# Hashed attention with the scores computed twice: once for the row maximum, once transposed for the product with V

## Chip, cores, metric

One Trainium2 chip (trn2), one core of it. The metric is the time of one execution on the device in microseconds (us), lower is better. Engines are named as in the profile: PE (TensorE), PEld (its weight loads), DVE (VectorE), ACT (ScalarE), POOL (GpSimd), SP (SyncE, which here only issues DMAs; SPq is its queue).

## What is computed

```python
# attention: batch 2, 8 heads, seq 768, head_dim 64; proj is 64 x 6
q_bits = (q @ proj > 0);  k_bits = (k @ proj > 0)          # 6 hash bits each
mask = bucket(q_bits)[:, None] == bucket(k_bits)[None, :]
scores = where(mask, q @ k.T / 8, -1e9)
scores -= max(scores, axis=-1)
attn = exp(scores);  attn /= sum(attn, axis=-1) + 1e-9
x = attn @ v                                               # (1536 tokens, 512)
# then a dense layer with SoLU and layer norm (512 -> 1024 -> 512)
# then a mixture of 8 experts, one expert per token (512 -> 1024 -> 512)
```

The change touches the attention alone: 16 heads of 768 queries by 768 keys.

## The kernel before

**Precision.** The tensors are float32. A score is made of fp32r products: q and k are split in a high part (ACT, L1022 and L1023) and a low part, the remainder (POOL, L1230), and a score tile is the sum of A1·B1 (high·high and high·low, stacked on 128 partitions) and A2·B2 (low·high, and below it the hash rows). The hash rows are 12 rows a head, made of the signs of q·proj and k·proj (PE L444, then DVE L705) and scaled so that a pair of unequal buckets adds a huge negative number to its score. So the mask costs no instruction of its own. The four operands of a head are put together by ten SBUF to SBUF DMAs that SP issues (fill, L363 to L376), into two sets of buffers, c = 0 and 1, for even and odd heads.

**One head**, queries on partitions. For each of six query tiles j of 128 rows: PE computes the scores (L454, four matmuls of 384 columns into two PSUM banks, a "slot"; there are two slots), DVE takes the negated row maximum (L712) and from it the scale and the bias (L714, L716), and ACT writes the exponentials to SBUF and their row sum (L1017). After three tiles (a half w of the head) DVE takes the reciprocal of the three sums (L723, L725), and POOL multiplies the three 128x768 tiles by it (normalize, L1223). V's product needs the keys on partitions, so PE then transposes the half's 18 blocks of 128x128 (L464), in six groups of three, and ACT (L1029) and DVE (L735) copy these out of PSUM to PTb. Then PE computes V's product for the half (L477): V's 128x64 block is the stationary operand, and two runs of 192 queries go to partitions 0 to 63 and 64 to 127 of one bank. Each of these float32 matmuls stands in the trace as two records. DVE copies the result of a head into xT (attended, L740).

**Order.** Every engine's order is written out by hand in a function heads(i, left) that holds a pair of heads; pairs() runs it for the first pair, then in a hardware loop for pairs 1 to 5, then for the last two. Within it PE takes scores of head h+1 and h+2 between the transposes and products of head h. Beside the attention, each head also prepares one piece of the dense layer's weights: DMA to stg, multiplied by g_ln on DVE (L729), high part on ACT (L1033), low part on POOL (L1235).

**Around it.** The first two heads' scores and exponentials stand ahead of the loop. After the last head the dense layer runs (hidden, L498 to L500, on), then routing, then the experts (from about 530 us). Their first input is take(), which splits xT in high and low parts (ACT L1046, POOL L1240).

## Time and profile before

| | |
|---|---|
| time, median of 3 runs | 787.79 us (786.18 to 789.93) |
| the profiled execution: its own time, its span | 788.34 us, 786.5 us |
| PE busy, weight loads busy | 628.5 us (80%), 508.3 us (65%) |
| DVE, ACT, POOL busy | 423.3, 323.8, 272.4 us |
| mean granted clock of PE | 0.901 |

The span is the time from the first to the last instruction of the profiled execution. The granted clock is the share of TensorE's full speed (2.4 GHz) that it was given: 1.00 or 0.50 in any stretch, and something between in a mean.

### The profile page before, as it was taken

How to read it: one execution, taken by the hardware profiler on the slowest of the kernel's cores; microseconds unless marked ns; L12 is line 12 of the kernel's file. 1: busy time of each engine (PE TensorE's matmuls, PEld its weight loads, DVE VectorE, ACT ScalarE, POOL GpSimd, SP SyncE). 2: the span in 40 equal slices, each digit the busy share in tenths (PEclk: the TensorE clock that was granted, in tenths of full speed). 3: DMA queues.
4: the chain of work that ended last, by engine and by line, in shares of the span. 5: the costliest groups of instructions: out<-in, count | busy, mean ns of one | idle time of the engine just before them, and what ended most of it. 6: DMA issues, size and time to landing. Idle time of an engine off the chain costs nothing.

```text
span 786.5 us, 12094 instructions
## 1 busy us (share of the span) xinstructions
PE 628.5 (80%) x3574; PEld 508.3 (65%) x3575; DVE 423.3 (54%) x764; ACT 323.8 (41%) x531; POOL 272.4 (35%) x200
## 2 busy tenths in 40 slices
PE   0658686868777787777999999981089999999994
PEld 0446565656565666655888888861078878878883
DVE  2546666666757565714465656546333564646431
ACT  1445555555545455532222222233243455545520
POOL 2365556565656464532123232253400100000010
PEclk9779888898989898987999999995589999999998
DMA  4457834435252515001000000022661756566510
GB/s 132 119 134 210 240 106 96 119 71 143 63 151 56 156 43 135 24 1 70 38 1 0 0 0 0 1 62 112 230 239 43 247 176 206 186 214 211 176 30 26
DMA packets 39262, 83.86 MB, mean 107 GB/s; under 512 B 7485, under 2 KB 10429, under 8 KB 39232
## 3 DMA queue, kind: packets, MB, share of 16 engines
q1 hardware_dynamic: 31952, 72.30, 31.5%
q10 hardware_dynamic: 5040, 4.87, 2.4%
q0 software_dynamic: 2240, 6.31, 2.1%
q8 instruction: 17, 0.28, 0.1%
q14 instruction: 13, 0.11, 0.0%
HBM read 52.09 MB, written 12.35 MB: 82 GB/s over the span
## 4 chain that ended last, share of the span: by engine, by line
PE 61%; DVE 11%; issue 8%; ACT 6%; POOL 5%; SPq 4%; DMA 4%; ACTq 1%; DVEq 1%; POOLq 0%
PE PS L477 8%; PE PS L454 6%; PE PS L464 4%; PE PS L646 4%; PE PS L648 4%; PE PS L647 3%; PE PS L498 3%; PE PS L500 3%; PE PS L627 3%; PE PS L499 3%; PE PS L628 3%; PE PS L629 3%; PE PS L558 3%; PE PS L560 3%; PE PS L559 3%
## 5 line engine op out<-in xcount | busy, mean ns | idle before, releaser
L1223 POOL TENSOR_TENSOR at_P<-at_P,sb_rr 128x768 f32<-128x768 f32 x96 | 138.3, 1468 | 119.2 <-DVE sb_rr L725 119.2
L454 PE MATMUL PS<-at_B,at_A 128*128 128x384 f32 x384 | 105.1, 403 | 35.3 <-DMA at_B<-at_HB 19.0
L712 DVE TENSOR_REDUCE sb_nm<-PS 128x1 f32<-128x768 f32 x96 | 91.6, 954 | 75.2 <-PE PS L454 74.7
L464 PE MATMUL PS<-sb_cst,at_P 128*128 128x128 f32 x576 | 79.5, 286 | 54.3 <-ACT at_PT L1029 54.3
L1017 ACT ACTIVATE at_P<-PS,sb_nb,sb_sc 128x768 f32<-128x768 f32 x96 | 95.7, 1000 | 65.1 <-DVE sb_nb L716 65.1
L454 PEld LDWEIGHTS PS<-at_B,at_A 128*128 128x128 f32 x384 | 72.2, 216 | 57.8 <-ACT at_P L1017 23.6
L464 PEld LDWEIGHTS PS<-sb_cst,at_P 128*128 128x128 f32 x576 | 67.5, 144 | 62.4 <-ACT at_PT L1029 40.2
L941 DVE TENSOR_TENSOR at_W<-at_raw,at_W 128x2048 f32 (+1 forms) x30 | 68.0, 2290 | 70.6 <-ACT at_W L1093 67.9
L1314 POOL DMA_INDIRECT out<-at_yb,sb_to x16 | 15.8, 985 | 204.3 <-DVE at_yb L953 204.3
L1093 ACT ACTIVATE at_W<-at_raw 128x2048 f32 (+1 forms) x32 | 60.4, 1911 | 61.4 <-issue 32.8
L477 PE MATMUL PS<-at_PT,at_V 128*64 128x192 f32 x768 | 85.1, 381 | 0.7 <-DVE at_PT L735 0.7
L1029 ACT ACTIVATE at_PT<-PS 128x384 f32<-128x384 f32 x144 | 61.5, 488 | 39.9 <-PE PS L464 39.9
L477 PEld LDWEIGHTS PS<-at_PT,at_V 128*64 128x64 f32 x768 | 61.8, 163 | 23.9 <-issue 8.4
L1269 POOL TENSOR_TENSOR at_cn<-at_eb,sb_mv 128x1024 f32<-128x1024 f32 x12 | 22.7, 1894 | 108.0 <-DVE sb_mv L763 108.0
L646 PE MATMUL PS<-at_W,at_hTh 128*128 x128 | 51.5, 402 | 5.0 <-DVE at_hTl L972 4.8
L627 PE MATMUL PS<-at_W,at_xsh 128*128 x128 | 52.6, 411 | 3.2 <-DVE at_xsl L945 3.2
L628 PE MATMUL PS<-at_W,at_xsh 128*128 x128 | 51.0, 399 | 0.0
L629 PE MATMUL PS<-at_W,at_xsl 128*128 x128 | 50.9, 398 | 0.0
L648 PE MATMUL PS<-at_W,at_hTl 128*128 x128 | 50.0, 391 | 0.0
L647 PE MATMUL PS<-at_W,at_hTh 128*128 x128 | 49.9, 390 | 0.0
L498 PE MATMUL PS<-at_wsp,at_xch 128*128 128x512 f32 x96 | 41.2, 430 | 7.3 <-POOL at_xcl L1240 7.3
L735 DVE COPY at_PT<-PS 128x384 f32<-128x384 f32 x48 | 26.6, 554 | 34.2 <-PE PS L464 34.2
(145 smaller groups left out, 1062.8 us busy)
## 6 DMA issues: line engine op xcount, KB each, us to landing
at_raw<-w SPq DMA_DIRECT2D x32, 1024.0 KB, 5.5
at_A<-at_H SPq DMA_DIRECT2D x32, 192.0 KB
at_B<-at_H SPq DMA_DIRECT2D x32, 192.0 KB
rows_by_expert<-at_empty SPq DMA_DIRECT2D x19, 257.0 KB, 6.4
at_XS<-rows_by_expert ACTq DMA_DIRECT2D x17, 256.0 KB, 2.6
at_stg<-w_solu SPq DMA_DIRECT2D x16, 256.0 KB, 3.3
at_R<-qT SPq DMA_DIRECT2D x8, 384.0 KB, 3.3
at_R<-kT SPq DMA_DIRECT2D x8, 384.0 KB, 4.2
```

The costliest lines, as they stand in the source:

```text
L454: m = mm(slot(j)[:, g, :], a[c][:, j * P:(j + 1) * P], b[c][:, g * HALF:(g + 1) * HALF], start=(a is A1), stop=(a is A2))
L464: m = pe.transpose(PS[:, T0 + kt % 3, j * P:(j + 1) * P], Pr[c][w][j][:, kt * P:(kt + 1) * P], ident)
L477: m = mm(PS[g * D:(g + 1) * D, PVB, w * QQ:(w + 1) * QQ], V[c][:, kt, :], PTb[w][:, kt, g * QQ:(g + 1) * QQ], start=(kt == 0), stop=(kt == ...
L627: mm(PS[:, g, :], xsh[:, x_k], W[:, high], start=(k == 0), stop=False)
L628: mm(PS[:, g, :], xsh[:, x_k], W[:, low], start=False, stop=False)
L629: m = mm(PS[:, g, :], xsl[:, x_k], W[:, high], start=False, stop=(k == KB - 1))
L646: mm(PS[:, 4 + c, :], hTh[:, h_f], W[:, high], start=(f == 0), stop=False)
L647: mm(PS[:, 4 + c, :], hTh[:, h_f], W[:, low], start=False, stop=False)
L648: m = mm(PS[:, 4 + c, :], hTl[:, h_f], W[:, high], start=False, stop=(f == FB - 1))
L712: dve.tensor_reduce(nm[:, col], slot(j), AX.XY, ALU.max, negate=True).then_inc(s_nm, 1)
L1017: fn(Pr[c][w][j % UT].rearrange("p (g n) -> p g n", g=2), slot(j), ACT.Exp, bias=nb[:, col], scale=sc[:, col], accum_out=sm[:, col]).then_ ...
L1223: pool.tensor_tensor(p, p, rr[:, col].broadcast_to([P, S]), ALU.mult).then_inc(s_norm, 1)
```

## The change

The scores of a head are computed in two forms.

1. leading(h, j), queries on partitions, six tiles: one product of the high parts with the hash rows stacked below (76 partitions, two matmuls of 384 columns a tile instead of four). DVE takes the negated row maximum as before (maximum), and that is all that is done with these scores.
2. maxima zeroes the maxima of rows without a partner, turn_maxima transposes the six columns of a head on PE, and place_maxima (DVE) writes them, less their sign, into six rows of A1 against rows of ones in B1.
3. products(h, kt), keys on partitions, six tiles of 128 keys: A1 and B1 (102 partitions: high parts, hash rows, maxima) and A2 and B2 (128 partitions: the two mixed products), for each half g of the queries into its own PSUM bank. So the maximum is already subtracted, and ACT's exponential (128x384, a constant scale, no bias, no sum) writes PT in the form that V's product reads. The transposes, their copies out of PSUM and POOL's multiplications are gone.
4. The row sums: POOL adds up the six PT tiles (add, five instructions a head), and sums multiplies the total by ones on PE, which leaves the sum in all 64 partitions. DVE takes 1/(sum + 1e-9) of 128x384 values (inverse) and scales V's product by it (attended). One more column in PT and V's product (385 instead of 384) carries a small term, mu, that is added to it.

V's product runs in two parts of three key tiles, (0, 1, 2) behind a head's own products and (3, 4, 5) in the middle of the next head. There are four sets of operands instead of two, filled three heads ahead (fill, still ten DMAs a head; at the start ACT issues half of them); R and HB are double. The scaling of the dense layer's weights by g_ln moves from DVE to ACT. The hardware loop over pairs becomes sixteen heads written out. The rows of zeros that SP writes to HBM in one run after the first pair now go two a head.

The core of the diff:

```diff
-QQ = UQ // 2
+SETS = 4
+ROWS1 = D + BITS
+MAXROW = 96
+ROWS = MAXROW + TILES
...
+        (PT,), w = many("PT", w, 1, KT * 2 * (HALF + 1))
+        PT = PT.rearrange("p (k g q) -> p k g q", k=KT, g=2)
+        w = (w + 7) // 8 * 8
+        acc, w = many("acc", w, 2, S)
+        (rec,), w = many("rec", w, 1, HALF)
...
+        STB, PVB, RB = 4, 6, 7
...
+            def fill(h):
+                sp.wait_ge(s_high, 2 * (h // 2) + 2)
+                sp.wait_ge(s_bits, h // 2 + 1)
+                wait(sp, s_st, 2 * KT * (h - SETS + 1))
+                for n in range(2):
+                    fill_1(sp, h, n)
+                sp.wait_ge(s_low, h // 2 + 1)
+                for n in range(2):
+                    fill_2(sp, h, n)
+            def load_v(h):
+                wait(sp, s_rb, h - 1)
+                sp.dma_start(V[h % 2], vP[h:h + 1].rearrange("o p (k d) -> p (o k) d", k=KT)).then_inc(ld_v[h % 2], 16)
...
+            def leading(h, j):
+                t, _, _ = set_of(h)
                 if j == 0:
-                    wait(pe, ld_f[c], FILL * p + FILL)
-                wait(pe, s_exp, 6 * h + j - 1)
-                for a, b in ((A1, B1), (A2, B2)):
+                    ready_1(pe, h)
+                wait(pe, s_nm, TILES * h + j - 1)
+                for g in range(2):
+                    m = mm(slot(h, j)[:, g, :], A1[t][0:ROWS1, j * P:(j + 1) * P],
+                           B1[t][0:ROWS1, g * HALF:(g + 1) * HALF], start=True, stop=True)
+                m.then_inc(s_slot, 1)
+            def turn_maxima(h):
+                pe.wait_ge(s_mm, h + 1)
+                m = pe.transpose(PS[0:TILES, RB, 0:P], mm_[:, h % 2 * TILES:(h % 2 + 1) * TILES], ident)
+                m.then_inc(s_mt, 1)
+            def products(h, kt):
+                t, _, _ = set_of(h)
+                if kt == 0:
+                    ready_2(pe, h)
+                    pe.wait_ge(s_mc, h + 1)
+                at_k = slice(kt * P, (kt + 1) * P)
+                for g in range(2):
+                    at_g = slice(g * HALF, (g + 1) * HALF)
+                    wait(pe, s_exp, 2 * (KT * h + kt) + g - 1)
+                    mm(PS[:, STB + g, 0:HALF], B1[t][0:ROWS, at_k], A1[t][0:ROWS, at_g], start=True, stop=False)
+                    mm(PS[:, STB + g, 0:HALF], B2[t][:, at_k], A2[t][:, at_g],
+                       start=False, stop=True).then_inc(s_st, 1)
+            def values(h, kts):
+                pe.wait_ge(s_exp, 2 * (KT * h + kts[-1]) + 2)
+                if kts[0] == 0:
+                    pe.wait_ge(ld_v[h % 2], 16 * (h // 2) + 16)
+                    wait(pe, s_fin, h)
+                for kt in kts:
                     for g in range(2):
-                        m = mm(slot(j)[:, g, :], a[c][:, j * P:(j + 1) * P], b[c][:, g * HALF:(g + 1) * HALF],
-                               start=(a is A1), stop=(a is A2))
-                m.then_inc(s_slot, 1)
-            def transposes(h, c, w, kts):
-                for kt in kts:
-                    if kt == 0:
-                        wait(pe, s_norm, 3 * (2 * h + w) + 3)
-                    wait(pe, *(evac_count(kt - 3, h, w) if kt >= 3 else evac_count(kt + 3, h - 1 + w, 1 - w)))
-                    for j in range(UT):
-                        m = pe.transpose(PS[:, T0 + kt % 3, j * P:(j + 1) * P],
-                                         Pr[c][w][j][:, kt * P:(kt + 1) * P], ident)
-                    m.then_inc(s_tr, 1)
-            def values(h, c, p, w):
-                wait(pe, *evac_count(ON_ACT[w][-1], h, w))
-                wait(pe, *evac_count(ON_DVE[w][-1], h, w))
-                if w == 0:
-                    wait(pe, ld_v[c], 16 * p + 16)
-                    wait(pe, s_pvev, h)
-                for kt in range(KT):
-                    for g in range(2):
-                        m = mm(PS[g * D:(g + 1) * D, PVB, w * QQ:(w + 1) * QQ], V[c][:, kt, :],
-                               PTb[w][:, kt, g * QQ:(g + 1) * QQ],
+                        m = mm(PS[g * D:(g + 1) * D, PVB, 0:HALF + 1], V[h % 2][:, kt, :], PT[:, kt, g, :],
                                start=(kt == 0), stop=(kt == KT - 1))
                 m.then_inc(s_pv, 1)
+            def sums(h):
+                pe.wait_ge(s_acc, (KT - 1) * (h + 1))
+                wait(pe, s_rec, 3 * h - 1)
+                for g in range(2):
+                    m = mm(PS[g * D:(g + 1) * D, RB, 0:HALF], cst[:, C_ONE:C_ONE + D],
+                           acc[h % 2][:, g * HALF:(g + 1) * HALF], start=True, stop=True)
+                m.then_inc(s_rb, 1)
...
+            for h in range(HEADS):
+                for kt in range(KT):
+                    ahead = (h + 1, kt + TILES - 2) if kt < 2 else (h + 2, kt - 2)
+                    if ahead[0] < HEADS:
+                        leading(*ahead)
+                    products(h, kt)
+                    if kt == 2:
+                        if h + 1 < HEADS:
+                            wait(pe, s_rec, 3 * h - 4)
+                            pe.wait_ge(s_bits, min(PAIRS, 2 + (h + 1) // 2))
+                            turn_maxima(h + 1)
+                        if h > 0:
+                            values(h - 1, (3, 4, 5))
+                            if h + 1 < HEADS:
+                                pe.wait_ge(s_mc, h + 2)
+                            sums(h - 1)
+                values(h, (0, 1, 2))
+                if h % 2 == 0 and h // 2 + 2 < PAIRS:
+                    wait(pe, s_rec, 3 * h - 1)
+                    hashes(h // 2 + 2, RB)
+            hidden(0, 0, 0, True)
+            values(HEADS - 1, (3, 4, 5))
+            sums(HEADS - 1)
+            hidden(0, 0, 1, True)
...
+            def maximum(h, j):
+                col = h % 2 * TILES + j
+                dve.wait_ge(s_slot, TILES * h + j + 1)
+                dve.tensor_reduce(nm[:, col:col + 1], slot(h, j), AX.XY, ALU.max, negate=True).then_inc(s_nm, 1)
+            def maxima(h):
+                cols = slice(h % 2 * TILES, (h % 2 + 1) * TILES)
+                dve.wait_ge(s_nm, TILES * h + TILES)
+                wait(dve, s_mt, h - 1)
+                dve.scalar_tensor_tensor(out=mm_[:, cols], in0=nm[:, cols], scalar=BIG / 2, in1=nm[:, cols],
+                                         op0=ALU.is_lt, op1=ALU.mult).then_inc(s_mm, 1)
+            def place_maxima(h):
+                dve.wait_ge(s_mt, h + 1)
+                dve.tensor_tensor(A1[h % SETS][MAXROW:ROWS, :].rearrange("p (j q) -> p j q", j=TILES),
+                                  PS[0:TILES, RB, 0:P].unsqueeze(1).broadcast_to([TILES, TILES, P]),
+                                  ident[0:TILES, 0:TILES].unsqueeze(2).broadcast_to([TILES, TILES, P]),
+                                  ALU.mult).then_inc(s_mc, 1)
+            def inverse(h):
+                dve.wait_ge(s_rb, h + 1)
+                dve.tensor_copy(mu[:, h % 2:h % 2 + 1], PS[:, PVB, HALF:HALF + 1]).then_inc(s_rec, 1)
+                dve.tensor_scalar(rec, PS[:, RB, 0:HALF], EPS, None, ALU.add).then_inc(s_rec, 1)
+                dve.wait_ge(s_rec, 3 * h + 2)
+                dve.reciprocal(rec, rec).then_inc(s_rec, 1)
+            def attended(h):
+                p, c = h // 2, h % 2
+                dve.wait_ge(s_rec, 3 * h + 3)
                 for g in range(2):
-                    m = dve.tensor_copy(
-                        xT[c * D:(c + 1) * D, ds(i * S, S)].rearrange("p (w g q) -> p w g q", w=2, g=2)[:, :, g, :],
-                        PS[g * D:(g + 1) * D, PVB, 0:UQ].rearrange("p (w q) -> p w q", w=2))
-                m.then_inc(s_pvev, 1)
+                    mine = slice(g * D, (g + 1) * D)
+                    m = dve.scalar_tensor_tensor(
+                        out=xT[c * D:(c + 1) * D, p * S + g * HALF:p * S + (g + 1) * HALF], in0=PS[mine, PVB, 0:HALF],
+                        scalar=mu[mine, c:c + 1], in1=rec[mine, :], op0=ALU.add, op1=ALU.mult)
+                m.then_inc(s_fin, 1)
...
+            for h in range(HEADS):
+                if h + 1 < HEADS:
+                    maximum(h + 1, TILES - 2)
+                    maximum(h + 1, TILES - 1)
+                    maxima(h + 1)
+                if h % 2 == 1 and h // 2 + 2 < PAIRS:
+                    hash_bits(h // 2 + 2, RB)
+                if h + 2 < HEADS:
+                    maximum(h + 2, 0)
+                if h + 1 < HEADS:
+                    place_maxima(h + 1)
+                if h > 0:
+                    inverse(h - 1)
+                if h + 2 < HEADS:
+                    maximum(h + 2, 1)
+                if h > 0:
+                    attended(h - 1)
+                if h + 2 < HEADS:
+                    maximum(h + 2, 2)
+                    maximum(h + 2, 3)
+            inverse(HEADS - 1)
+            attended(HEADS - 1)
...
+            def weights_of(h, kt, g):
+                act.wait_ge(s_st, 2 * (KT * h + kt) + g + 1)
+                if h > 0 and g == 0:
+                    act.wait_ge(s_pv, 2 * h - 1 if kt < 3 else 2 * h)
+                    act.wait_ge(s_acc, (KT - 1) * (h - 1) + max(kt, 1))
+                fn(PT[:, kt, g, 0:HALF], PS[:, STB + g, 0:HALF], ACT.Exp, scale=SCALE).then_inc(s_exp, 1)
...
+            for h in range(HEADS):
+                weights_of(h, 0, 0)
+                weights_of(h, 0, 1)
+                if h % 2 == 1 and h // 2 + 2 < PAIRS:
+                    high_parts(h // 2 + 2)
+                weights_of(h, 1, 0)
+                weights_of(h, 1, 1)
+                weights_scaled(h)
+                weights_of(h, 2, 0)
+                weights_of(h, 2, 1)
+                if h == HEADS - 1:
+                    act.wait_ge(s_rows0, 16 * SLOTS)
+                weights_high(h)
+                for kt in (3, 4, 5):
+                    weights_of(h, kt, 0)
+                    weights_of(h, kt, 1)
...
+            def add(h, kt):
+                total = acc[h % 2].rearrange("p (g q) -> p g q", g=2)
+                pool.wait_ge(s_exp, 2 * (KT * h + kt) + 2)
+                if kt == 1:
+                    wait(pool, s_rb, h - 1)
+                else:
+                    pool.wait_ge(s_acc, (KT - 1) * h + kt - 1)
+                pool.tensor_tensor(total, PT[:, 0, :, 0:HALF] if kt == 1 else total, PT[:, kt, :, 0:HALF],
+                                   ALU.add).then_inc(s_acc, 1)
...
+            for h in range(HEADS):
+                if h % 2 == 1 and h // 2 + 2 < PAIRS:
+                    low_parts(h // 2 + 2)
+                add(h, 1)
+                weights_low(h)
+                for kt in range(2, KT):
+                    add(h, kt)
```

## Rows read from the trace of the kernel before

**Rows 1.** Page: busy us (share of the span) and instructions of each engine.
```profile
PE 628.5 (80%) x3574; PEld 508.3 (65%) x3575; DVE 423.3 (54%) x764; ACT 323.8 (41%) x531; POOL 272.4 (35%) x200
```

**Rows 2.** Windows: stretch, length, engines' busy us (instructions), clock, DMA share, GB/s.
```profile
76.70:117.70 41.00, 31.98 (x228) 25.45 (x224) 24.96 (x57) 22.02 (x46) 23.27 (x17) 0.88 0.66 179
117.70:158.50 40.80, 31.62 (x228) 24.77 (x228) 25.98 (x57) 22.01 (x46) 23.42 (x17) 0.87 0.41 103
...
381.00:520.00 139.00, 137.64 (x710) 116.02 (x710) 86.11 (x140) 38.17 (x54) 38.41 (x32) 1.00 0.00 0
```

**Rows 3.** Waits in three turns, 76.7 to 199.4: total, times, longest.
```profile
POOL at_P L1223 <- DVE sb_rr L725: 42.5, 13, 5.4
...
PE PS L464 <- ACT at_PT L1029: 22.7, 6, 5.5
```

**Rows 4.** Groups by form, same turns: count, busy us, mean ns, idle before.
```profile
L1223 POOL TENSOR_TENSOR at_P<-at_P,sb_rr 128x768 f32<-128x768 f32 x37 | 53.3, 1466 | 42.5 <-DVE sb_rr L725 42.5
L454 PE MATMUL PS<-at_B,at_A 128*128 128x384 f32 x144 | 38.7, 395 | 4.8 <-ACT at_P L1017 4.7
L1017 ACT ACTIVATE at_P<-PS,sb_nb,sb_sc 128x768 f32<-128x768 f32 x36 | 35.9, 1000 | 16.3 <-DVE sb_nb L716 16.3
L712 DVE TENSOR_REDUCE sb_nm<-PS 128x1 f32<-128x768 f32 x36 | 34.4, 954 | 20.6 <-PE PS L454 20.5
L477 PE MATMUL PS<-at_PT,at_V 128*64 128x192 f32 x288 | 32.2, 384 | 0.0
L464 PE MATMUL PS<-sb_cst,at_P 128*128 128x128 f32 x216 | 30.2, 288 | 22.7 <-ACT at_PT L1029 22.7
...
L1029 ACT ACTIVATE at_PT<-PS 128x384 f32<-128x384 f32 x54 | 23.0, 488 | 12.9 <-PE PS L464 12.9
L1230 POOL TENSOR_TENSOR at_R<-at_R,at_H 128x768 fp32r<-128x768 f32 x6 | 10.8, 1827 | 5.1 <-ACT at_H L1022 5.1
...
L740 DVE COPY at_xT<-PS 64x384 f32 x12 | 6.7, 556 | 1.9 <-PE PS L477 1.6
...
L1022 ACT ACTIVATE at_H<-at_R 128x768 fp32r<-128x768 f32 x3 | 2.5, 832 | 0.0
```

**Rows 5.** Timeline of TensorE in one turn: start us, us, engine, line.
```profile
140.64 0.65 PEld L454 LDWEIGHTS PS<-at_B,at_A 128*128 128x128 f32 x4 [0.28 <-issue]
140.64 0.97 PE L454 MATMUL PS<-at_B,at_A 128*128 128x384 f32 x4
...
145.10 1.82 PEld L477 LDWEIGHTS PS<-at_PT,at_V 128*64 128x64 f32 x24 [0.25 <-ACT at_PT L1029]
```

**Rows 6.** Groups by form, whole span: the three sizes of reciprocal.
```profile
L725 DVE RECIPROCAL sb_rr<-sb_se 128x3 f32<-128x3 f32 x32 | 5.6, 176 | 1.1
...
L757 DVE RECIPROCAL sb_rs<-sb_se 128x1 f32<-128x1 f32 x12 | 2.0, 164 | 0.4
...
L868 DVE RECIPROCAL sb_r<-sb_r 128x12 f32<-128x12 f32 x1 | 0.2, 228 | 0.3 <-ACT sb_r L1123 0.3
```

**Rows 7.** Timeline 368 to 373 us: a short VectorE instruction beside a GpSimd one.
```profile
370.45 1.90 POOL L1269 TENSOR_TENSOR at_cn<-at_eb,sb_mv 128x1024 f32<-128x1024 f32 x1
370.59 1.77 DVE L768 TENSOR_TENSOR sb_var_all<-sb_var_all,sb_rs 128x1 f32<-128x1 f32 x1
```

**Rows 8.** Windows around TensorE's long wait in a turn.
```profile
150.00:152.50 2.50, 0.00 (x0) 0.00 (x0) 2.47 (x4) 0.80 (x2) 1.29 (x1) 1.00 0.96 358
...
153.70:157.10 3.40, 3.40 (x17) 2.31 (x17) 1.79 (x4) 2.10 (x6) 0.12 (x1) 0.50 0.00 0
```

**Rows 9.** Timelines: first ten fills' first and last; first scores; second hidden tile.
```profile
12.07 1.20 SPq L371 DMA_DIRECT2D at_A<-at_H  x2
...
19.09 0.71 SPq L376 DMA_DIRECT2D at_B<-at_HB  x1
...
21.12 2.93 PE L454 MATMUL PS<-at_B,at_A 128*128 128x384 f32 x8 [12.76 <-DMA at_B<-at_HB]
...
370.75 0.77 PE L498 MATMUL PS<-at_wsp,at_xch 128*128 128x512 f32 x1 [4.73 <-POOL at_xcl L1240]
```

427 lines of the change are left out of this document (140 added, 287 removed).

## Prediction, made before the changed kernel was run

> **What bounds the kernel now.** I read the page first, then windows by stage, the waits, the groups by form and the timeline of one turn. The page shows no engine full: PE 80%, DVE 54%, ACT 41%, POOL 35% of the span [rows 1]. The stages tell why that mean misleads. From 381 to 520 us, in the dense layer, PE is busy 137.6 of 139 us at clock 1.00: nothing there is touched. In the attention, one turn of the loop (two heads) takes 40.8 us, in which PE is busy 31.6, DVE 26.0, POOL 23.4, ACT 22.0, at a mean clock of 0.87 [rows 2]. So a head takes 20.4 us and nothing is saturated: it is a chain that goes round the engines. The waits give its links [rows 3]: POOL waits 42.5 us in three turns for the reciprocal, and PE waits 22.7 us, in pieces up to 5.5 us, for ACT's copies of the transposes. These idle stretches cost a second time: behind 2.5 us without a matmul, PE ran 3.4 us at clock 0.50 [rows 8]. What the change is worth is therefore the new length of a head, against 20.4.
>
> **What goes.** Per head, from three turns [rows 4]: 36 transposes (30.2/6 = 5.0 us of PE), nine copies on ACT and three on DVE, six multiplications on POOL (53.3/6 = 8.9 us), and the step maximum, bias, exponential, reciprocal, multiply, transpose, copy. The new order has no such round between a head's scores and its weights, except for the maxima, which are a head ahead.
>
> **What PE has now, full clock.** Four score matmuls take 0.65 us of loads and 0.97 us to their last end, so 0.163 each and a tail of 0.32 [rows 5]. leading: 12 x 0.163 = 1.95; products: 24 x 0.163 = 3.9. V's product streams 12 x 385 columns where 24 x 192 were streamed; half of it took 1.82 [rows 5], so three key tiles take 1.9, with the gap of 0.28 ahead of the next matmul 2.2, twice 4.4. sums is a sixth of V's product, 0.64. Turning the maxima 0.15; the hash products of a pair stream 384 columns four passes deep side by side, so as sums 0.64 with tail and gap, half a pair: about 0.5. V's product and sums are float32, and their two column halves run side by side as now. Sum 11.5, against about 14 before.
>
> **The pace of products.** Each bank is written by two matmuls, read by an exponential, and written again. Two matmuls 0.33, tail 0.32, exponential, 0.06 to PE's next. The exponential of 128x384 is not in the trace: a copy of that form takes 488 ns, an exponential of twice that 1000 [rows 4]. I take 0.53. So 1.24 us a key tile, while PE has 0.98 of work in it. ACT has six pairs of exponentials and three to four other instructions, some 7.5 us a head: not a bound, but the high parts of q and k (2 x 0.83 [rows 4]) stand between two exponentials in every odd head: 0.6 on average.
>
> **DVE.** Six maxima x 0.954 [rows 4], maxima 0.2, place_maxima about 0.95 (768 columns, as L712), hash bits 0.35, mu 0.15, the addition of 1e-9 from PSUM 0.6 (as L740), attended 2 x 0.57 [rows 4], and the reciprocal of 128x384. This one is the unknown. Its three sizes took 164, 176 and 228 ns for 1, 3 and 12 columns [rows 6]: 5.8 ns a column over both steps, so 0.164 + 383 x 0.0058 = 2.4 us. The lower bound is the rate of the other DVE rows, 1.04 ns a column: 0.56 us. Upper bound 3.3, if the slope at few columns flatters it. I take 2.4. DVE then has 11.7 us a head.
 The slope here is nearer to 5.6 cycles; by the page's figure the stall below is 0.8 us longer and the forecast some 11 us later.
>
> **POOL.** Five additions a head of two full 128x768 tiles. The nearest row is the low part, 1827 ns [rows 4], not the multiplication by a broadcast column, 1466; 9.1 us (7.3 by the other). With the low parts 1.8 and the weights' low part about 1.25: 12.2 us. The additions end some 8 to 11 us behind the point T below, sums needs them at about 14: hidden, if a head takes over 13 us.
>
> **SP.** Still ten fills a head: the first ten went out from 12.07 to 19.80 us, 0.77 each [rows 9]. 7.7 us a head, plus three loads and for ten heads two rows of zeros: under 11, and asked for more than a head ahead. No cost.
>
> **A full head, walked.** T = 0 is the end of sums(h-1). What is queued on DVE behind it decides: maximum(h+2, 1) stands behind inverse, and leading(h+2, 3) on PE waits for that maximum. DVE: tail 0.32, mu, addition, reciprocal with starts between 3.3, maximum 0.97: 4.6. PE meanwhile has only key tiles 3 and 4, until 2.2: it stalls 2.4 us. Key tile 5 until 5.6; V's product waits for attended (4.6 + 1.15 = 5.75) and ends at 8.0; hash products 0.5; key tiles 0 and 1, 2.5, high parts 0.6; key tile 2 and the turned maxima 1.1; V's product 2.2; sums 0.64. Sum 15.6. place_maxima is ready about 14.0, sums at 14.9: hidden, with 0.9 us to spare.
> The clock: 2.4 us of stall is near the 2.5 us that half clock followed [rows 8], but the other gaps of a head are 0.3 us or less. I take a half-clock stretch of 3.4 us in half of the heads; it does half of its work, so 1.7 us are lost each time: 0.8 a head. A full head: 16.4 us.
>
> **The sum.** First scores: operands for the maximum need no low parts (2 x 1.83 earlier) and three DMAs issued by SP beside three by ACT, not ten: about 13 us instead of 21.1 [rows 9]. Six maxima, turning and placing: products of head 0 at 22, some 3 us for head 2's operands: 25. Head 0 has no sums and no stall (six key tiles 7.4, V's product 2.2, turning 0.15, hash products 1.1): 10.9. Heads 1 to 13: 13 x 16.4 = 213. Heads 14 and 15 have no leading tiles and so no stall for them (7.4, V's product twice 4.4, sums 0.64, turning 0.15, and 1.1 in which V's product waits for attended): 2 x 13.7 = 27.4. That is 276.5. Then the tail: one half of the hidden tile (12 matmuls of 512 columns at the rate of the score matmuls) 2.6, V's product 2.2, sums 0.64, inverse and attended 4.8, take(), two thirds of L1022 on ACT and of L1230 on POOL, 2.0: the second hidden tile starts at 289 instead of 370.7 [rows 9]. 82 us less. The rest is unchanged: 788.3 - 82 = 706 for the profiled execution's own time (span 786.5 and 1.8 around it); the median was 0.5 under that execution, so 706 again.
>
> **Rivals.**
> **A, the division is cheap** (0.56 us): the stall goes from 2.4 to 0.55, and with it the half clock; 13 x (1.85 + 0.6) and 2 in the rest, so 34 less: 672. For it: only sizes of up to 12 columns are seen. Against it: both steps of the slope agree.
> **B, DVE and POOL block each other.** For it: L768, of 128x1, took 1.77 us and ended with a POOL instruction of 1.90 that had started before it [rows 7]. POOL will be busy three quarters of a head. maxima reads two operands in SBUF as L768 does, and the reciprocal reads and writes SBUF. Waiting for the addition in progress is up to 1.8 us, 0.9 on average, at each; on the path in the reciprocal, half so in maxima: 1.4 a head, with POOL's own delay up to 2.5. 13 x 1.4 to 13 x 2.5: 724 to 739. Against: POOL has 2 to 4 us of room.
> The Trainium skill ("SBUF — State Buffer", SBUF: two separate sides) says so: VectorE with two SBUF inputs, or in a 2-port mode, and GpSimd lock each other out for a whole instruction. The row agrees.
> **C, slower than before: PE never regains its clock.** Its work between exponentials is 0.98 of every 1.24 us, then a stall. If this pace is too low for the granted clock all along, the head's 11.5 us of PE become about 22, with what is left of the stall 23.4: 7 x 13, 8 and 15 at the ends, 114 more: 820. It decides from some 72% of the attention at half clock (82/114). Against it: after the half-clock stretch, which PE filled, the clock came back [rows 8], and at half clock PE is always full.
> The Trainium skill ("TensorE: Matmul & The Clock Gate", A second HAM failure mode: psum-queue depth-cycling) tells of a kernel that cycles through PSUM banks, idles briefly between groups and oscillates between the clocks; the oscillation is in my 0.8, the steady low clock is C.
>
> **How the numbers follow.** Forecast 0.50 (690 to 722), A 0.20 (655 to 690), B 0.22 (722 to 745), C 0.04, and 0.04 for something else that eats the gain, a product of V whose two halves no longer overlap (12 x 385 columns one after another: 4 us a head) or operands that come late. The range takes A and B: 666 to 742. Under 0.5% a measurement here can hardly tell from no change, about 4 us. Faster 0.94, same 0.01, slower 0.05.
>
> **What would show it.** One RECIPROCAL of 128x384 a head, at 2.4 us; PE waiting about 2.4 us for DVE's L712 once a head; no PE wait on ACT over 0.7 us but in odd heads; POOL's additions at 1.8 us and never waited for by sums; maxima stretched where POOL works; a head of 15.5 to 16.5 us; clock in the attention 0.85 to 0.95; second hidden tile at about 289 us. It is wrong if the stall in PE is elsewhere (sums behind POOL, products behind place_maxima), or if the head's length is set by ACT.

## The result and the profile after

| | before | changed |
|---|---|---|
| time, median of 4 runs on one chip | 787.21 us (786.18 to 789.93) | 710.52 us (709.01 to 714.1) |
| ratio, 95% interval | | 0.9027 (0.8985 to 0.907) |
| the profiled execution: own time, span, mean clock | 788.34, 786.5 us, 0.901 | 709.71, 707.6 us, 0.925 |

The change made the kernel 9.7% faster. The forecast was 706 us, in a range of 666 to 742.

The page of the changed kernel: busy time of the engines, the chain that ended last, two groups.

```profile
PE 598.6 (85%) x2886; PEld 440.4 (62%) x2887; DVE 400.0 (57%) x525; ACT 259.0 (37%) x403; POOL 268.5 (38%) x188
...
PE 70%; DVE 13%; issue 4%; DMA 3%; ACT 3%; POOL 2%; SPq 2%; ACTq 1%; DVEq 0%; POOLq 0%
...
L1242 POOL TENSOR_TENSOR at_acc<-at_acc,at_PT 128x768 f32<-128x768 f32 x64 | 107.6, 1681 | 14.8 <-ACT at_PT L1027 10.3
...
L754 DVE RECIPROCAL at_rec<-at_rec 128x384 f32<-128x384 f32 x16 | 40.9, 2553 | 0.5
```

Against [rows 1], PE lost 30 us of work, DVE 23, ACT 65, POOL 4, and none of them was full. The gain of 79 us in the span is thus mostly idle time. Line numbers have moved: leading is L472, turn_maxima L478, products L491 and L492, values L503, sums L512, the maximum L730, maxima L737, place_maxima L743, inverse L751 (mu), L752 (1e-9) and L754 (reciprocal), attended L762, the exponential L1027, high_parts L1036, low_parts L1231, add L1242, take L1252, hidden L533 to L535.

I cut the attention at each start of L751, which stands right behind sums, so that a stretch is one head. Windows of the changed kernel, with the columns of [rows 2]: three heads, one idle stretch of PE in the third, and what follows it.

```profile
116.02:130.10 14.08, 12.44 (x66) 7.78 (x67) 10.94 (x14) 6.26 (x14) 11.30 (x9) 1.00 0.94 235
130.10:146.09 15.99, 13.42 (x74) 8.05 (x75) 11.56 (x14) 7.61 (x16) 11.28 (x7) 1.00 0.46 123
146.09:161.73 15.64, 14.00 (x66) 8.60 (x67) 10.93 (x13) 6.37 (x14) 11.28 (x9) 0.89 0.95 231
148.56:150.17 1.61, 0.00 (x1) 0.00 (x1) 1.61 (x3) 0.50 (x2) 1.47 (x2) 1.00 1.00 217
150.50:153.90 3.40, 3.40 (x12) 2.00 (x12) 2.57 (x4) 0.98 (x2) 3.11 (x3) 0.50 1.03 307
```

A head takes 14.08 us, or 15.99 with the hash products and high parts of a pair, at full clock. With one stretch of half clock (3.4 us at 0.50, as in [rows 8]) it is 1.6 longer: the third row is a short head. From the first start of L751, 52.64, to the thirteenth, 242.61, there are 12 heads of 15.83 us on average, against 20.4 [rows 2]: seven of the short kind and five of the long one, with seven half-clock stretches among them.

The waits from 100 to 250 us, some ten heads:

```profile
DVE sb_nm L730 <- PE PS L472: 20.6, 9, 3.5
PEld PS L472 <- DVE sb_nm L730: 20.2, 11, 2.0
DVE sb_mu L751 <- PE PS L512: 17.8, 10, 1.8
PE PS L472 <- DVE sb_nm L730: 16.4, 10, 1.6
...
PE PS L491 <- ACT at_PT L1027: 3.5, 4, 0.9
```

POOL's wait for a reciprocal and PE's for ACT's copies [rows 3] are gone. PE now has one long wait a head, ten times 1.6 us, for a maximum. The timeline shows where it comes from. Below are first PE's rows, then DVE's, of the changed kernel around 116 us; sums of one head ends at 115.97, the point T of the prediction.

```profile
115.16 0.81 PE L512 MATMUL PS<-at_acc,sb_cst 128*64 128x384 f32 x4
115.91 0.62 PE L472 MATMUL PS<-at_B,at_A 76*128 76x384 f32 x2
...
120.10 0.62 PE L472 MATMUL PS<-at_B,at_A 76*128 76x384 f32 x2 [1.64 <-DVE sb_nm L730]
...
121.36 2.16 PE L503 MATMUL PS<-at_PT,at_V 128*64 128x385 f32 x12
...
129.24 0.81 PE L512 MATMUL PS<-at_acc,sb_cst 128*64 128x384 f32 x4
```

```profile
116.02 0.16 DVE L751 COPY sb_mu<-PS 128x1 f32<-128x1 f32 x1 [1.80 <-PE PS L512]
116.10 0.55 DVE L752 TENSOR_SCALAR at_rec<-PS 128x384 f32<-128x384 f32 x1
116.68 2.55 DVE L754 RECIPROCAL at_rec<-at_rec 128x384 f32<-128x384 f32 x1
119.15 0.89 DVE L730 TENSOR_REDUCE sb_nm<-PS 128x1 f32<-128x768 f32 x1
119.97 1.23 DVE L762 SCALAR_TENSOR_TENSOR at_xT<-PS,sb_mu,at_rec 64x384 f32<-64x384 f32 x2
```

DVE sits idle for 1.80 us until sums is done. Then mu, the addition and the division hold it for 3.1 us. The scores of tile 1, which ended at 116.53, wait behind them for their maximum, and PE, which needs their banks for tile 3, runs out of work at 118.46.

Groups by form of the changed kernel, 100 to 250 us: mean ns behind the busy time.

```profile
L1242 POOL TENSOR_TENSOR at_acc<-at_acc,at_PT 128x768 f32<-128x768 f32 x40 | 67.2, 1681 | 9.7 <-ACT at_PT L1027 7.2
L730 DVE TENSOR_REDUCE sb_nm<-PS 128x1 f32<-128x768 f32 x57 | 53.0, 944 | 22.2 <-PE PS L472 20.6
L1027 ACT ACTIVATE at_PT<-PS 128x384 f32<-128x384 f32 x114 | 50.1, 491 | 85.6 <-PE PS L492 85.3
```

The additions on POOL are somewhat shorter than the low parts of [rows 4], the maximum is as it was, and the exponential of 128x384 takes as long as a copy of that form did.

### The profile page after: what moved, and what is told of

It is laid out like the page before. It is cut to its first block, busy times and chain, and to the rows that moved or that the text cites. A ratio compares the mean times of both kernels' runs of the same rounds, so it can differ in the third digit from the quotient of the medians.

```text
span 707.6 us, 9729 instructions
## 1 busy us (share of the span) xinstructions
PE 598.6 (85%) x2886; PEld 440.4 (62%) x2887; DVE 400.0 (57%) x525; ACT 259.0 (37%) x403; POOL 268.5 (38%) x188
## 4 chain that ended last, share of the span: by engine, by line
PE 70%; DVE 13%; issue 4%; DMA 3%; ACT 3%; POOL 2%; SPq 2%; ACTq 1%; DVEq 0%; POOLq 0%
PE PS L503 11%; DVE at_rec L754 6%; PE PS L664 5%; PE PS L666 4%; PE PS L665 4%; PE PS L645 4%; PE PS L646 3%; PE PS L647 3%; PE PS L491 3%; PE PS L533 3%; PE PS L535 3%; PE PS L578 3%; PE PS L534 3%; PE PS L472 3%; PE PS L580 3%
## 5 line engine op out<-in xcount | busy, mean ns | idle before, releaser
L1027 ACT ACTIVATE at_PT<-PS 128x384 f32<-128x384 f32 x192 | 84.6, 491 | 135.2 <-PE PS L492 134.3
L730 DVE TENSOR_REDUCE sb_nm<-PS 128x1 f32<-128x768 f32 x96 | 89.2, 947 | 43.7 <-PE PS L472 41.3
L1242 POOL TENSOR_TENSOR at_acc<-at_acc,at_PT 128x768 f32<-128x768 f32 x64 | 107.6, 1681 | 14.8 <-ACT at_PT L1027 10.3
L503 PE MATMUL PS<-at_PT,at_V 128*64 128x385 f32 x384 | 80.0, 557 | 3.1 <-DVE at_xT L762 2.7
L472 PE MATMUL PS<-at_B,at_A 76*128 76x384 f32 x192 | 58.6, 394 | 28.0 <-DVE sb_nm L730 23.3
L491 PE MATMUL PS<-at_A,at_B 102*128 102x384 f32 x192 | 73.9, 385 | 9.5 <-ACT at_PT L1027 9.5
L472 PEld LDWEIGHTS PS<-at_B,at_A 76*128 76x128 f32 x192 | 34.4, 205 | 54.9 <-DVE sb_nm L730 31.8
L492 PE MATMUL PS<-at_A,at_B 128*128 128x384 f32 x192 | 67.3, 350 | 0.0
L503 PEld LDWEIGHTS PS<-at_PT,at_V 128*64 128x64 f32 x384 | 29.1, 152 | 40.4 <-issue 34.4
L491 PEld LDWEIGHTS PS<-at_A,at_B 102*128 102x128 f32 x192 | 37.5, 195 | 26.6 <-ACT at_PT L1027 20.4
L533 PE MATMUL PS<-at_wsp,at_xch 128*128 128x512 f32 x96 | 39.9, 416 | 6.2 <-POOL at_xcl L1252 6.2
L754 DVE RECIPROCAL at_rec<-at_rec 128x384 f32<-128x384 f32 x16 | 40.9, 2553 | 0.5
```

The lines of the kernel that those rows point to most:

```text
L472: m = mm(slot(h, j)[:, g, :], A1[t][0:ROWS1, j * P:(j + 1) * P], B1[t][0:ROWS1, g * HALF:(g + 1) * HALF], start=True, stop=True)
L491: mm(PS[:, STB + g, 0:HALF], B1[t][0:ROWS, at_k], A1[t][0:ROWS, at_g], start=True, stop=False)
L503: m = mm(PS[g * D:(g + 1) * D, PVB, 0:HALF + 1], V[h % 2][:, kt, :], PT[:, kt, g, :], start=(kt == 0), stop=(kt == KT - 1))
L730: dve.tensor_reduce(nm[:, col:col + 1], slot(h, j), AX.XY, ALU.max, negate=True).then_inc(s_nm, 1)
L754: dve.reciprocal(rec, rec).then_inc(s_rec, 1)
L1027: fn(PT[:, kt, g, 0:HALF], PS[:, STB + g, 0:HALF], ACT.Exp, scale=SCALE).then_inc(s_exp, 1)
```

## The experiments

The theory tested by e1, e2, e3 and e10 is that of the prediction: the chain on DVE behind sums costs a stall of PE in each head, and this stall some of the clock. e5, e6 and e9 test the place of the high and low parts, e7 the load of GpSimd, e4 and e8 another engine for the division. "PE busy" and "clock" below are from windows from 62 to 238 us, 176 us inside the attention; the last column is the number of stretches of half clock in it, 3.4 us each where nothing else is said.

| kernel | median us | ratio to before (95%) | PE busy, clock | half-clock stretches |
|---|---|---|---|---|
| changed | 710.52 | 0.9027 (0.8985 to 0.907) | 153.3, 0.94 | 6 |
| e1, short division | 671.68 | 0.8546 (0.8513 to 0.8579) | 170.2, 1.00 | 0 |
| e2, division split | 703.10 | 0.8949 (0.8918 to 0.898) | 152.4, 0.98 | 2 |
| e5, high parts late | 698.70 | 0.8885 (0.8852 to 0.8917) | 156.0, 0.94 | 6 |
| e7, short additions | 711.00 | 0.9053 (0.9015 to 0.909) | 153.4, 0.94 | 6 |
| e3, sums first | 673.90 | 0.8559 (0.8521 to 0.8596) | 169.6, 1.00 | 0 |
| e4, exp(-ln) on ACT | 700.03 | 0.8903 (0.8851 to 0.8954) | 156.2, 0.97 | 3 |
| e6, e3 and e5 | 693.13 | 0.8794 (0.8755 to 0.8834) | 162.0, 0.92 | 4 of 6.8 us |
| e8, e4 and e5 | 700.27 | 0.8912 (0.8848 to 0.8976) | 155.0, 0.95 | 5 |
| e9, e3, head 1 as in e5 | 676.06 | 0.8598 (0.8572 to 0.8624) | 169.9, 0.99 | the end of one |
| e10, maximum first | 727.34 | 0.925 (0.9221 to 0.928) | 147.8, 0.91 | 9 |

The kernel before took 785.88 us beside the first four (e1, e2, e5, e7), 787.09 beside the next four, 786.90 beside the last two.

### e1_short_division: what the division costs

```diff
-                dve.reciprocal(rec, rec).then_inc(s_rec, 1)
+                dve.reciprocal(rec[:, 0:12], rec[:, 0:12]).then_inc(s_rec, 1)
```

Only 12 of 384 columns are divided; all waits and all other work stay.

> The changed kernel with the reciprocal cut from 384 to 12 columns (the other 372 are left as sums, so the output is not scaled there): 2.55 us become about 0.23. Theory 1 (VectorE's chain behind sums, up to attended, sets the length of a head): PE's waits of 1.64 us for L730 go, V's product follows key tile 5 at once, a head falls from 15.7 to about 13.4 us, and the time from 710 to about 678 (675 to 683). Theory 2 (the division is beside the path, PE's own work and the exponentials set the length): within 3 us of 710. Theory 3 (POOL takes over as soon as the division is short): a head of about 14.5, time 692 to 700, with PE's L512 waiting for POOL.

Measured: 39 us under the changed kernel, 3 more than the range of theory 1 allowed (675 to 683); theories 2 and 3 are out. Two heads of e1, cut at L751:

```profile
105.22:117.56 12.34, 12.34 (x66) 7.72 (x67) 8.66 (x14) 6.26 (x14) 11.31 (x9) 1.00 0.93 228
117.56:131.66 14.10, 13.24 (x74) 7.84 (x75) 9.24 (x14) 7.61 (x16) 11.27 (x7) 1.00 0.71 175
```

They take 12.34 and 14.10 us instead of 14.08 and 15.99: 1.8 a head at full clock, and there is no half-clock stretch left, which is 0.95 more (seven short and five long heads at full clock are 14.88 on average in the changed kernel, and 15.83 was measured). Twelve heads take 156.9 us instead of 190.0, 33 less; 6 more come between the thirteenth start of L751 and the second hidden tile. In the short head PE has no idle time at all.

### e2_division_split: the same work in another order

```diff
-                dve.reciprocal(rec, rec).then_inc(s_rec, 1)
+                dve.reciprocal(rec[:, 0:HALF // 2], rec[:, 0:HALF // 2])
+            def inverse_rest(h):
+                dve.reciprocal(rec[:, HALF // 2:HALF], rec[:, HALF // 2:HALF]).then_inc(s_rec, 1)
...
                     maximum(h + 2, 1)
                 if h > 0:
+                    inverse_rest(h - 1)
                     attended(h - 1)
```

> The changed kernel with the reciprocal in two halves of 192 columns and maximum(h+2, 1) between them; the same work in another order. Theory 1a (two waits end together: leading's for this maximum and V's product's for attended): the wait of PE for L730 falls from 1.64 to about 0.4 us, a wait for DVE's L762 of about the same size appears ahead of V's product, and the time stays at 710, within 3 us. Theory 1b (the queue position of this one maximum is the whole cost): 1.3 us a head less, time 692 to 696.

Measured: 7 us under the changed kernel. The waits of e2, 100 to 250 us:

```profile
PE PS L503 <- DVE at_xT L765: 13.1, 10, 1.3
PEld PS L472 <- DVE sb_nm L730: 10.6, 15, 0.8
```

The stall is moved, as expected: less for the maximum, and 1.3 us a head for attended, which V's product needs. At full clock a head is no shorter (14.25 and 16.05 us against 14.08 and 15.99). I had expected no change within 3 us, and missed: two short waits in the place of one of 1.6 us left two half-clock stretches instead of six. Four times 1.6 is 6.4 of the 7 us. All four executions of e2 had a mean clock of 0.946 to 0.948, those of the changed kernel 0.922 to 0.935. By that count it was the shape of the stall, and not its sum, that made the difference, through the clock; why two short waits have fewer such stretches behind them is not shown.

### e10_maximum_first: the whole division behind the maximum

```diff
-                if h > 0:
-                    inverse(h - 1)
                 if h + 2 < HEADS:
                     maximum(h + 2, 1)
                 if h > 0:
+                    inverse(h - 1)
                     attended(h - 1)
```

> The changed kernel with maximum(h+2, 1) moved ahead of inverse(h-1) in VectorE's queue, nothing else. Theory 1a (leading's wait and V's product's wait for attended end together): PE's wait for L730 of 1.64 us goes, but the division starts about 0.6 to 0.9 us later, so V's product waits some 2.5 us for L762 and a head is 0.3 to 0.9 us longer: 712 to 722. Theory 1b (that maximum's place is the cost): 1.6 us a head less, 685 to 691.

Measured: 17 us slower than the changed kernel, 5 more than theory 1a allowed (712 to 722), and theory 1b is out. The waits of e10, 100 to 250 us:

```profile
DVE sb_nm L730 <- PE PS L472: 43.4, 17, 3.5
PEld PS L503 <- issue: 43.3, 89, 2.7
...
PE PS L503 <- DVE at_xT L762: 21.5, 9, 2.4
```

PE's wait for the maximum is gone and a longer one, 2.4 us, stands before V's product, with a stretch of half clock in nearly every head. A short head at full clock takes 14.80 us instead of 14.08, as theory 1a had it; what it had not counted are the added half-clock stretches (9 instead of 6 in the 176 us). The remedy that suggests itself, to serve the waiting engine first, made it worse: the division only delays another thing that PE needs.

### e3_sums_first: both waits taken away

PE computes sums(h-1) behind key tile 1 and not between V's product and key tile 3; DVE does the division behind the last maxima of the next head, and V's product of head h-1 follows it while DVE divides.

```diff
+                    if kt == 1:
+                        pe.wait_ge(s_bits, min(PAIRS, 2 + (h + 1) // 2))
+                        if h > 0:
+                            sums(h - 1)
                     if kt == 2:
...
                             values(h - 1, (3, 4, 5))
-                            if h + 1 < HEADS:
-                                pe.wait_ge(s_mc, h + 2)
-                            sums(h - 1)
...
+                if h % 2 == 1 and h // 2 + 2 < PAIRS:
+                    hash_bits(h // 2 + 2, RB)
                 if h + 1 < HEADS:
                     maximum(h + 1, TILES - 2)
                     maximum(h + 1, TILES - 1)
                     maxima(h + 1)
-                if h % 2 == 1 and h // 2 + 2 < PAIRS:
-                    hash_bits(h // 2 + 2, RB)
-                if h + 2 < HEADS:
-                    maximum(h + 2, 0)
-                if h + 1 < HEADS:
-                    place_maxima(h + 1)
                 if h > 0:
                     inverse(h - 1)
                 if h + 2 < HEADS:
+                    maximum(h + 2, 0)
                     maximum(h + 2, 1)
                 if h > 0:
                     attended(h - 1)
+                if h + 1 < HEADS:
+                    place_maxima(h + 1)
```

mu is copied in attended instead of inverse, V's load waits for V's product instead of sums, and some counts that PE waits for are adapted. No work is left out.

> The same work as the changed kernel in another order: on PE sums(h-1) directly behind products(h, 1), ahead of the turned maxima and the second part of V's product; on DVE the reciprocal directly behind maxima(h+1), so that it runs beside V's product, then maximum(h+2, 0) and (h+2, 1), attended (with mu), place_maxima. Theory (it is the place of the division in DVE's queue, not DVE's total of 11.7 us): PE's stall goes although the division is whole; heads of 12.6 and 14.4 us, as with the short division, with up to 0.8 us of waiting for GpSimd's last addition in every second head; time 674 to 685. Rival (DVE is too full for any order): stall at another place of DVE's queue, time 700 or more.

Measured: 673.90 us, 14.4% under the kernel before and 37 us under the changed one, at the lower edge of what was expected. It is the fastest full version here. Its windows, cut at sums:

```profile
100.35:114.22 13.87, 12.77 (x67) 7.61 (x66) 12.09 (x15) 8.50 (x19) 13.17 (x9) 1.00 0.70 169
114.22:127.53 13.31, 13.31 (x73) 7.86 (x74) 11.20 (x13) 5.57 (x13) 9.40 (x6) 1.00 0.85 221
```

PE is busy for the whole of the second and for 92% of the first, at full clock throughout, though each division still takes 2553 ns. DVE does more per microsecond than before (11.2 to 12.1 us of work a head). What cost the time was the division's place in the order, in DVE's queue and behind sums on PE, and not DVE's load; which of the two moves does how much was not tried apart. PE now bounds the second kind of head. In the first kind it waits 1.10 us once, ahead of sums: the profile names no releaser, but the addition on GpSimd that sums needs ends at 114.12 (rows below, under rival B) and sums starts at 114.22. So GpSimd, which was hidden before, now costs about a microsecond in every second head (five such waits between 20 and 250 us). The row of this wait in the timeline of PE:

```profile
114.22 0.87 PE L512 MATMUL PS<-at_acc,sb_cst 128*64 128x384 f32 x4 [1.10 <-issue]
```

### e7_short_adds: is GpSimd hidden?

```diff
+                n = HALF if kt < 3 else 8
-                pool.tensor_tensor(total, PT[:, 0, :, 0:HALF] if kt == 1 else total, PT[:, kt, :, 0:HALF],
-                                   ALU.add).then_inc(s_acc, 1)
+                pool.tensor_tensor(total[:, :, 0:n], PT[:, 0, :, 0:n] if kt == 1 else total[:, :, 0:n],
+                                   PT[:, kt, :, 0:n], ALU.add).then_inc(s_acc, 1)
```

The row sums lack most of key tiles 3 to 5.

> The changed kernel with GpSimd's additions of key tiles 3 to 5 cut to 8 of 384 columns of each half (so the row sums lack half of the tiles): GpSimd has some 4.5 us less work a head. Theory (GpSimd is hidden, 2 us or more of room, and it doesn't slow VectorE): within 3 us of 710, PE never waits for GpSimd in either. Rival (the additions delay the exponentials or VectorE's work through the ports): 8 us or more are gained.

Measured: POOL's work from 62 to 238 us falls from 122.3 to 74.4 us, and the time stays, as expected (711.00 against 710.52), with the same PE busy time, clock and number of half-clock stretches. GpSimd is hidden in the changed kernel; the rival, 8 us or more, is out.

### e5_high_late: high and low parts further back

```diff
-                if h % 2 == 1 and h // 2 + 2 < PAIRS:
-                    high_parts(h // 2 + 2)
                 weights_of(h, 1, 0)
...
                 weights_high(h)
+                if h % 2 == 1 and h // 2 + 2 < PAIRS:
+                    high_parts(h // 2 + 2)
```

and in the same way low_parts behind weights_low on GpSimd.

> The changed kernel with the high parts of the next pair on ScalarE, and the low parts on GpSimd, behind weights_high and weights_low instead of ahead of key tile 1. Theory (my walk: they cost PE a wait in odd heads; and in head 1 they wait for the fills of heads 2 and 3, which held PE for 3.7 us): odd heads 0.9 us shorter, six of them, and head 1 about 4 us shorter: 710 falls to 700 to 703. Rival (the head is set by VectorE's chain alone, and the wait in odd heads is taken out of that chain's slack): only head 1 gains, 705 to 707.

Measured: 12 us under the changed kernel, a little more than the 700 to 703 that were expected. The first L751 starts at 45.69 us instead of 52.64: 7.0. The rest is in the odd heads. Two heads of e5:

```profile
62.02:78.67 16.65, 14.95 (x74) 8.58 (x75) 11.56 (x15) 7.73 (x16) 10.16 (x8) 0.90 0.58 163
78.67:92.73 14.06, 12.41 (x66) 7.75 (x67) 11.02 (x14) 6.37 (x14) 12.76 (x8) 1.00 0.77 189
```

The first has a half-clock stretch; without its 1.6 us it is 15.05 against 15.99: 0.9 less. Twelve heads take 185.8 us instead of 190.0, five of them being of this kind. So the high parts did stand between PE and its next exponential, and the fills that they wait for cost 7 us at the start.

### e6_sums_first_high_late: e3 and e5 together

> The order of e3_sums_first and that of e5_high_late together. The gains are at different places (the stall for DVE in every head; the high parts ahead of key tile 1 in odd heads and the wait for fills in head 1), so they should add: 12 us less than e3_sums_first, 662 to 673. Rival: GpSimd, which then does the low parts behind the first addition, ends its additions later than sums now wants them, and the two together gain little over e3_sums_first.

Measured: 19 us slower than e3, where 12 us less had been expected, and worse than the rival, by which little was gained: a clear miss, though the rival had named its cause. The waits of e6, 20 to 250 us:

```profile
POOL at_wsp L1247 <- ACT at_wsp L1044: 28.9, 15, 3.5
...
PE PS L512 <- issue: 17.5, 6, 3.5
```

In e3, sums comes about a key tile and a V's product earlier, so the additions have little room (in the first of the two windows of e3 above POOL is busy 13.17 of 13.87 us). GpSimd now waits for weights_low's operand first, the additions end late, and PE waits for them in sums, up to 3.5 us; the clock falls to 0.92. The profile calls this wait "issue"; that it is for the additions is read from the timeline, where one ends at 120.90 us and sums starts at 121.00. Two gains that are real each by itself were not to be added.

### e9_sums_first_head1_late: e3, with e5's edit in head 1 alone

> e3_sums_first, with the high and low parts of pair 2 (in head 1) behind weights_high and weights_low, the other pairs as in e3. Theory: the wait of head 1 for the fills of heads 2 and 3 was worth 7 us in e5_high_late, about half of it comes back because sums(1) now waits for GpSimd as in e6_sums_first_high_late: 3 to 7 us under e3_sums_first, 667 to 671. Rival: the fills themselves are late, and head 1 only waits at another place: 673 to 675.

Measured: 676.06 us, no gain over e3 (673.90), so the theory (667 to 671) is out, and the time is 1 us above the rival's 673 to 675. sums(0) starts at 41.71 us instead of 44.06, sums(1) at 58.63 instead of 59.85, sums(2) at 74.33 instead of 73.17: the lead is lost in two heads, in the first of them by PE's wait in sums, as in e6. The wait of e9 between 36 and 62 us:

```profile
PE PS L512 <- issue: 3.5, 1, 3.5
```

### e4_ln_exp and e8_ln_exp_high_late: the division on ScalarE

1/(sum + 1e-9) is computed as exp(-ln(sum + 1e-9)) by two ACT instructions behind weights_high; DVE has neither the addition nor the reciprocal. e8 has e5's edit as well.

```diff
-                dve.tensor_scalar(rec, PS[:, RB, 0:HALF], EPS, None, ALU.add).then_inc(s_rec, 1)
-                dve.wait_ge(s_rec, 3 * h + 2)
-                dve.reciprocal(rec, rec).then_inc(s_rec, 1)
...
+                fn(rec, PS[:, RB, 0:HALF], ACT.Ln, bias=epsb[:, :]).then_inc(s_rec, 1)
+                act.wait_ge(s_rec, 2 * h + 1)
+                fn(rec, rec, ACT.Exp, scale=-1.0).then_inc(s_rec, 1)
```

> The changed kernel with 1/(sum + 1e-9) taken on ScalarE as exp(-ln(sum + 1e-9)), two activations of 128x384 behind weights_high, instead of the addition and the reciprocal on VectorE (3.1 us of it a head). If both functions lie in one table: as with the short division, 671 to 678. If each needs its own table (1.28 us a load in the rows of before, two loads a head, ahead of key tile 3's exponentials): some 2.6 us a head come back, 705 to 720.

> e4_ln_exp with the order of e5_high_late. If the tables need no switch: 12 us less than e4_ln_exp, 660 to 666, the shortest of all, because DVE has 3.1 us less a head and sums is asked for later than in e6. If they do, it follows e4_ln_exp, 12 us below it at most.

Measured: e4 is 10 us under the changed kernel, 5 less than the lowest that was expected with table loads; e8 is the same as e4, which its expectation left open (at most 12 us less). Groups of ACT in e4, 100 to 250 us:

```profile
L1033 ACT ACT_TABLE_LOAD x10 | 12.8, 1283 | 0.2
L1035 ACT ACT_TABLE_LOAD x10 | 12.8, 1283 | 0.2
...
L1033 ACT ACTIVATE at_rec<-PS,sb_epsb 128x384 f32<-128x384 f32 x10 | 5.8, 581 | 3.8 <-PE PS L514 3.8
L1035 ACT ACTIVATE at_rec<-at_rec 128x384 f32<-128x384 f32 x10 | 5.2, 522 | 0.1
```

Each head pays two loads of a function table, 2.6 us, and 1.1 us of arithmetic on ACT, more than the 2.55 us of the division. It still gains: the maximum that PE needs no longer stands behind the division, and no wait of PE for L733 (the maximum here) is among the long ones. But PE now waits for the exponentials (17.5 us in ten heads, up to 2.0 each). e5's edit, worth 12 us alone, is worth nothing here. The traces show where its gain goes, and not why: the first mu is copied 3.7 us earlier in e8 than in e4 (48.61 against 52.28), but the twelve heads from there take 185.5 us instead of 177.9, with 5 half-clock stretches instead of 3 in the 176 us.

## Why the prediction was right

**The new chain.** Right in its place, its cause and, nearly, its sizes. It named maximum(h+2, 1) behind inverse as what PE would wait for, with V's product behind attended next. Walked against measured, from T = 115.97:

| | walk | measured |
|---|---|---|
| reciprocal of 128x384 | 2.4 | 2.55 |
| maximum(h+2, 1) done | T + 4.6 | T + 4.07 |
| PE's stall | 2.4 | 1.64 |
| V's product starts | T + 5.75 | T + 5.39 |
| a key tile at the pace of the exponentials | 1.24 | 1.20 |
| V's product, three key tiles, alone | 2.2 | 2.16 |
| a head at full clock | 15.6 | 14.88, mean of seven of 14.08 and five of 15.99 |
| lost to the clock, a head | 0.8 | 0.95 |
| a head | 16.4 | 15.83 |

The stall came out 0.76 short: DVE's chain ended 0.5 earlier than walked, with no gaps between its instructions, and PE had work until T + 2.49 instead of T + 2.2. V's product had 0.16 us to spare behind attended, which ended at 121.20, and did not wait for it; the walk had it wait 0.15. The forecast named one stretch of half clock in every second head; there were 7 in the twelve heads, at 1.6 us each. That it would be half of the heads was a choice and not derived, and it was made for a stall of 2.4 us: in e10, where PE does wait 2.4 us, there were 9 stretches in some ten heads. So this term came out near because the stall was shorter than walked, by luck in part.

**The reciprocal.** It was the largest unknown, between 0.56 and 3.3 us. The slope over three short rows [rows 6] gave 2.4; 2553 ns less the 164 of one column are 6.2 ns a column, against 5.8 taken.
**Rival A**, the cheap division, did not happen, but e1 is nearly that kernel (0.23 us of division instead of 0.56): the prediction priced it at 34 us less, it measured 39 less. Part of the gap is in the sum, which gives back 0.6 a head for the clock where the walk had charged 0.8 and the runs show 0.95.

**Rival B**, DVE and POOL blocking each other, did not happen: 711 and not 724 to 739. But its mechanism is half there. All 16 reciprocals took 2552 to 2555 ns, with GpSimd at work beside them (that of 116.68 ran beside L1247 until 117.46 and then beside L1242), so this reciprocal, with one operand, in SBUF, isn't blocked. maxima, which has two, took 165 or 166 ns in all 16 heads, and each time GpSimd was idle when it started; the closest case of the changed kernel:

```profile
141.12 0.17 DVE L737 SCALAR_TENSOR_TENSOR sb_mm<-sb_nm 128x6 f32<-128x6 f32 x1
141.18 3.60 POOL L1231 TENSOR_TENSOR at_Ro<-at_Ro,at_H 128x768 fp32r<-128x768 f32 x2 [3.38 <-ACT at_H L1036]
```

In e3 the same instruction meets a busy GpSimd:

```profile
110.61 3.51 POOL L1242 TENSOR_TENSOR at_acc<-at_acc,at_PT 128x768 f32<-128x768 f32 x2
...
113.26 0.88 DVE L737 SCALAR_TENSOR_TENSOR sb_mm<-sb_nm 128x6 f32<-128x6 f32 x1
```

It takes 0.88 us and ends at 114.14, with the addition that ends at 114.12; so in five heads of e3. This agrees with the rule of the Trainium skill ("SBUF — State Buffer", SBUF: two separate sides), which speaks of two SBUF inputs, as far as these two instructions show it. The prediction was right to give B a small price; its sentence that the reciprocal would be blocked was the wrong part of it, and "maxima stretched where POOL works" was not seen in the changed kernel because maxima never started beside an instruction of GpSimd.

**Rival C**: the clock came back after each stretch. From 62 to 238 us it was 0.94, not near 0.5.

**POOL.** Additions 1681 ns, the first of a head 1546, against 1827 taken. Never waited for by sums (in the head that begins at 116.02 the last addition ends at 124.61, and sums starts at 129.24), and hidden (e7), as said. e3 and e6 show how near the edge it is once sums comes earlier.

**The start: the term that was mis-sized.** "No cost" for the fills was wrong in head 1, and the clock there was not counted. The first L751, right behind the first sums, started at 52.64; the forecast's own steps put it at 25 + 10.9 + 7.1 = 43, where 7.1 is the part of the walked head from its first products (T + 8.5 of 15.6) to the next T. First scores came at 14.45 (13 forecast) and products of head 0 at 27.56 (25). Then, in the changed kernel:

```profile
44.37 1.58 ACT L1036 ACTIVATE at_H<-at_Re 128x768 fp32r<-128x768 f32 x2 [2.70 <-DMA at_B<-at_H]
...
46.37 0.69 PE L491 MATMUL PS<-at_A,at_B 102*128 102x384 f32 x1 [3.69 <-ACT at_PT L1027]
```

ACT's high_parts for the third pair of heads waits for the fills of heads 2 and 3, which read the buffer that it overwrites, and the exponentials stand behind it. PE waits 3.7 us and runs at clock 0.50 from there to 51.5, as it had from 14 to 31: 3.7 and half of 5.1 and of the 3.4 from 27.56 on are 7.9, about the 7.1 missing between 27.56 and 52.64. e5, which moves these high parts, starts its first L751 7.0 earlier. In steady state the fills cost nothing: from 100 to 250 us no long wait of PE or ACT is for a DMA.

**The sum.** The start came 9.6 later than forecast, twelve heads took 6.8 less, what lies from there to the second hidden tile 0.5 less: 2.3 over 289.

```profile
291.33 0.77 PE L533 MATMUL PS<-at_wsp,at_xch 128*128 128x512 f32 x1 [6.24 <-POOL at_xcl L1252]
```

From there to the end the changed kernel takes 416.3 us, the one before 415.7 [rows 9], as assumed. Two errors of 10 and 7 us cancelled: that the forecast of 706 came out nearer than its parts was luck.

**What the prediction did not see** is that the stall was a matter of order alone. It summed DVE's work, 11.7 us a head (its own terms add up to 11.5; 10.9 to 11.6 measured), took the queue as given, and did not ask whether the same work in another order would fill PE. e3 does so, but for 1.1 us in every second head, and is worth 37 us.

## What to carry to other kernels

When a long instruction enters a queue between two others that a second engine waits for, walk both waits: putting it behind either (e10), or half behind each (e2), moves the stall, and of the orders tried here only an earlier start of what feeds it (e3) takes it away. Before two gains are added, look at how much room the third engine has left by the first of them (e6: 19 us lost). A stall's price includes the clock behind it: here 1.6 us for each stretch of half clock, and a stall in two pieces had fewer of them. When a forecast comes out right, compare its parts too: here two wrong ones cancelled.

## What the runs showed of the hardware

- The reciprocal of 128x384 float32 took 2553 ns in the changed kernel and in e3, 6.2 ns a column beyond the first, and wasn't lengthened by GpSimd's work.
- A VectorE instruction with two operands in SBUF took 882 ns at most instead of 166 in e3, up to 1386 in e5 and 1452 in e6, each time where it met a GpSimd addition.
- Ln and Exp in alternation cost an ACT_TABLE_LOAD of 1283 ns at each switch, two a head.
- V's product with its two column halves side by side: six matmuls of 385 columns, 12 records, took 2.16 us (timeline at 121.36), 180 ns a record.
